# A fused attention and feed-forward kernel on one core: both products one item earlier, masks one item later, two row copies on ScalarE's queue

## What is computed

```python
for t in range(S):
    new_re = ar * S_re - ai * S_im
    new_im = ar * S_im + ai * S_re
    S_re, S_im = (new_re + kv, new_im)          # kv = outer(k_t, v_t)
    y[:, :, t] = einsum('bhd,bhde->bhe', q_t, S_re)
x = y as 3072 tokens of 384
h = x @ w_in;  x = (h * clip(h + 3, 0, 6) / 6) @ w_out          # 384 -> 2048 -> 384
h = x @ w_in2; out = (max(h, 0) + alpha * min(h, 0)) @ w_out2
```

## Time and profile before

| | |
|---|---|
| median of 3 runs (lowest, highest) | 1027.42 us (1025.89 to 1032.92) |
| the profiled execution: its time | 1026.65 us |
| its span, first to last instruction | 1024.7 us |
| mean granted TensorE clock | 0.986 of full speed |
| TensorE matmuls busy | 967.1 us, 94% of the span |
| VectorE busy | 599.4 us, 58% |
| ScalarE busy | 485.4 us, 47% |
| GpSimd busy | 263.2 us, 26% |

### The profile page before, as it was taken

One profiled execution on the slowest core, in us unless ns is written; L12 is line 12 of the kernel. 1 busy time (PEld: TensorE's weight loads), 2 busy tenths in 40 slices (PEclk: granted clock), 3 DMA queues, 4 the chain that ended last, 5 costly groups with the idle time before them and its releaser, 6 DMA issues.

```text
span 1024.7 us, 17083 instructions
## 1 busy us (share of the span) xinstructions
PE 967.1 (94%) x6498; PEld 869.2 (85%) x6498; DVE 599.4 (58%) x1088; ACT 485.4 (47%) x865; POOL 263.2 (26%) x235
## 2 busy tenths in 40 slices
PE   0799987999999999999999999999999999999997
PEld 0788877899999999999999998888888888888886
DVE  6767787778878878878772244453433433434332
ACT  7656666667677676777743453221221222212211
POOL 0000022222222222322222243333333333323332
PEclk9999988999999999999999999999999999999999
DMA  6752322333433333442221611001010010100000
GB/s 171 207 141 70 86 70 71 87 85 95 106 82 94 85 94 77 104 110 71 78 68 27 241 61 54 1 20 43 1 62 1 1 62 1 62 1 1 32 1 31
DMA packets 80930, 70.48 MB, mean 69 GB/s; under 512 B 32592, under 2 KB 78160, under 8 KB 80464
## 3 DMA queue, kind: packets, MB, share of 16 engines
q1 hardware_dynamic: 80208, 68.80, 24.7%
q10 hardware_dynamic: 640, 0.59, 0.3%
HBM read 40.90 MB, written 9.44 MB: 49 GB/s over the span
## 4 chain that ended last, share of the span: by engine, by line
PE 83%; SPq 5%; ACT 4%; DVE 4%; DMA 2%; issue 2%; DVEq 0%; ACTq 0%
PE op L1189 12%; PE op L1190 12%; PE hp L1190 12%; PE op L1191 12%; PE hp L1189 12%; PE hp L1191 11%; SPq L402 3%; PE yp L1177 3%; PE gp L1156 3%; SPq L405 2%; PE yp L1156 2%; DMA st<-prod 2%; PE gp L1184 2%; PE hp L1212 1%; PE tp L1165 1%
## 5 line engine op out<-in xcount | busy, mean ns | idle before, releaser
L524 POOL TENSOR_TENSOR g_lo<-gated,g_hi 128x384 fp32r<-128x384 f32 (+2 forms) x224 | 261.0, 1165 | 752.1 <-ACT g_hi L620 752.1
L620 ACT ACTIVATE g_hi<-gated 128x384 fp32r<-128x384 f32 (+2 forms) x224 | 123.3, 551 | 330.0 <-DVE gated L904 284.4
L900 DVE TENSOR_SCALAR gate<-hp,alpha_sb 128x512 f32<-128x512 f32 x96 | 72.1, 751 | 240.0 <-PE hp L1191 240.0
L889 DVE SCALAR_TENSOR_TENSOR gated<-gate,hp 128x384 f32<-128x384 f32 (+1 forms) x144 | 72.8, 506 | 125.3 <-ACT gate L613 125.0
L1189 PE MATMUL op<-g_hi,wb_hi 128*128 128x384 f32 (+1 forms) x384 | 129.3, 337 | 0.4 <-ACT out_sb L625 0.2
L1189 PE MATMUL hp<-x_hi,wa_hi 128*128 128x384 f32 (+1 forms) x384 | 126.0, 328 | 0.0
L613 ACT ACTIVATE gate<-hp,half 128x384 f32<-128x384 f32 (+1 forms) x144 | 77.2, 536 | 101.9 <-PE hp L1191 87.7
L1191 PE MATMUL op<-g_hi,wb_lo 128*128 128x384 f32 (+1 forms) x384 | 124.8, 325 | 0.0
L1190 PE MATMUL op<-g_lo,wb_hi 128*128 128x384 f32 (+1 forms) x384 | 124.7, 325 | 0.0
L1191 PE MATMUL hp<-x_hi,wa_lo 128*128 128x384 f32 (+1 forms) x384 | 123.7, 322 | 0.0
L1190 PE MATMUL hp<-x_lo,wa_hi 128*128 128x384 f32 (+1 forms) x384 | 123.6, 322 | 0.0
(11 more groups left out here) (110 smaller groups left out, 1704.1 us busy)
## 6 DMA issues: line engine op xcount, KB each, us to landing
st<-prod SPq DMA_DIRECT2D x92, 145.1 KB, 2.9
a_sb<-a_in SPq DMA_DIRECT2D x24, 288.0 KB, 4.0
qk_sb<-qk_in SPq DMA_DIRECT2D x24, 288.0 KB, 3.6
v_pad<-v_in SPq DMA_DIRECT2D x24, 192.0 KB, 3.8
x_raw<-x SPq DMA_DIRECT2D x6, 768.0 KB, 5.6
out<-out_sb SPq DMA_DIRECT2D x6, 768.0 KB, 4.0
st<-prod SPq DMA_DIRECT2D x96, 32.2 KB, 2.3
wa_raw<-w_in SPq DMA_DIRECT2D x6, 512.0 KB, 6.1
```

Of the source, the lines that this page charges most:

```text
L524: pool.tensor_tensor(g_lo[:, at, 0:wide], gated[:, at * UT:at * UT + wide], g_hi[:, at, 0:wide].bitcast(F32), ALU.subtract).then_inc(glo_d ...
L620: act.activation(g_hi[:, at, 0:wide], gated[:, at * UT:at * UT + wide], ACT.Copy).then_inc(ghi_done, 1)
L889: dve.scalar_tensor_tensor(out=gated[:, to], in0=gate[:, at], scalar=1.0, in1=hp[:, n % 2, 0:wide], op0=ALU.min, op1=ALU.mult).then_inc(ga ...
L900: dve.tensor_scalar(gate[:, at], hp[:, n % 2, 0:wide], 0.0, alpha_sb[:, m:m + 1], ALU.min, ALU.mult).then_inc(gate_done, 1)
```

## The change

The strings of the short slots change: `c` goes from the third item to the second, so that `forward` and `backward` stand together; `d` stays in the third and `e` and `g` join it from the fourth, so that both products stand in the third; `f` (masks) goes from the second item to the fourth, and `o` (outputs) from the third to the fourth, where `v` remains. `stack(c1)` on SyncE goes with `g` to the third item. For the chunks that a short slot prepares (and chunk 2), the two large row copies of the second product are issued on ScalarE's queue: in the fourth item, with `f`, behind `gate_of`, `copy_k` and `logs` of that item if it has them, and ahead of `inverses`. The function for this is there already, and serves chunks 0 and 1: it waits for `ends_set` and for the second product.

```diff
-SHORT = {6: ("a", "bf", "cdo", "egv", "hij", "kl"), 7: ("a", "bf", "cdo", "egv", "hi", "j", "kl")}
+SHORT = {6: ("a", "bc", "deg", "fov", "hij", "kl"), 7: ("a", "bc", "deg", "fov", "hi", "j", "kl")}
...
+def is_short(s):
+    return width(items_of(s)[-1] // MT_FF) == FIRST * CH
+
+def two_queues(c):
+    return c <= FIRST or is_short(c - 1)
...
# SyncE, in stack(c)
-                for to, rows in high_stack(c, 1) + ([] if c < FIRST else low_stack(c, 1)):
+                for to, rows in high_stack(c, 1) + ([] if two_queues(c) else low_stack(c, 1)):
...
# ScalarE, ahead of the loop over items
             inverses(3)
+            stack(2)
             gate_of(0)
...
# ScalarE, in the loop over items
+                if "f" in steps and c1 is not None and two_queues(c1):
+                    stack(c1)
                 if "v" in steps and c2 is not None:
                     inverses(c2)
```

More of the change, by code:

```diff
@@ L126, in places @@
         items = items_of(s)
-        plan = (SHORT if width(items[-1] // MT_FF) == FIRST * CH else LONG)[len(items)]
+        plan = (SHORT if is_short(s) else LONG)[len(items)]
         for steps, n in zip(plan, items):
```

## The result

| | before | changed |
|---|---|---|
| median | 1029.99 us (4 runs, 1025.89 to 1032.92) | 1039.65 us (4 runs, 1039.17 to 1042.63) |
| profiled execution, its span | 1026.65, 1024.7 us | 1039.17, 1037.5 us |
| mean granted clock | 0.986 | 0.984 |

The ratio (of the means; the medians differ by 9.7 us) is 1.0103, 95% interval 1.0056 to 1.015: slower by about 10.6 us. The forecast was no change, 1027.0 in a range from 1016 to 1036, with a chance of 0.1 for slower; it missed.

A forecast was written before the change was run, and what follows sets the result against it. TensorE's stops and low clock in slots 2 to 8 were taken as the bound: 143.8 us of work, 22.8 of stops and 7.5 of clock make 174.1 against 174.5, hence 1027.0 us, range 1016 to 1036.

The forecast's parts named there:

- The wait moves from the copies to the masks: Slots 2 to 8: TensorE stops mid-slot for VectorE's masks, about 2.2 us seven times, instead of for row copies.
- The wait for `leave` in slot 4: Slot 4, third item: TensorE's `output(16)` waits 2.5 us for `leave`, which now stands behind logs.
- The split that `high` feeds: Behind ScalarE's issues: TensorE wants this split two items later, so the delay costs nothing in slots without weight splits.
- VectorE's lag: VectorE starts phases behind TensorE's scores: 1 us on slots 3 to 5, 3 us on slot 6, 4 us in all.
- The clock: Slots 2 to 8: five of seven stops each cost 1.7 us of low clock, 8.5 less 1 hidden: 7.5 us.
- Rival B: The clock holds through the 2.2 us stops: less 7.5 us, 1019.5 us, chance 0.2.
- The start of slot 2: Ahead of item 0, ScalarE's `stack(2)` delays nothing: 0, bound 0 to 1.2 us.
- ScalarE's issues in slots with splits: Fourth item: two issues on ScalarE, 1.25 us a pair, would cost 1.25 to 3 us a slot without cover.
- Rival C: ScalarE's fourth-item wait and issues hold up VectorE's split and carry its lag over: 8 to 10 us, 1036 us, chance 0.14.
- phases more than 0.2 us behind the scores: Sign of Rival C at slot starts: VectorE starting phases this late delays ScalarE's waves and the second item's gate.
- The sum: Slots 2 to 8: work 143.8, stops 22.8 and clock 7.5 make 174.1 us against 174.5, no change.
- the signs named beforehand: Next profile: mask waits seven times, `leave` wait, PEclk 0.93 in most slots, slots 4 and 5 shorter, slot 8 longer.

The follow-up runs named there:

- e3: The changed kernel with the masks moved back to the second item, behind backward: 1025.52 us, ratio 0.9978 to the kernel before.
- e10: The kernel before with only masks, outputs and new_state moved to the fourth item, all copies on SyncE: 1045.47 us, ratio 1.0172.
- e11: The kernel before with backward and logs in the second item, both products in the third, all copies on SyncE: 1022.22 us, ratio 0.9945.
- e1: The changed kernel's order alone, with SyncE issuing all 12 row copies: 1041.6 us, ratio 1.0124 to the kernel before.
- e12: The changed kernel with ScalarE's two issues in the fifth item and chunk 2 all from SyncE: 1040.84 us, ratio 1.0126 to the kernel before.
- e5: e3 without the second queue, all twelve row copies on SyncE: 1020.4 us, ratio 0.9911 to the kernel before.
- e6: e3 with chunk 2's copies all issued from SyncE, without `stack(2)` on ScalarE: 1027.01 us, ratio 0.9976 to the kernel before.
- e2: The kernel before, order kept, with the two copies on ScalarE's queue in the fourth item, chunk 2's too: 1036.55 us, ratio 1.0081.

## Why the prediction was wrong, step by step

**The wait moves from the copies to the masks: right, its size partly by luck.** Forecast 16.3 us at the masks (2.3, 2.3, 1.4, 3.7 and three of 2.2); measured 16.0, with none in slot 4 and 2.95 in slot 3. In slot 8 both sides of the sum were late and the difference held: the masks ended 15.2 us behind the slot's start instead of 13.7, and TensorE arrived after 12.9 us instead of 11.4, most of it by the stop for `g_lo`. The copies left the path. That the masks are the harm is shown by e3 and e10, that the products' half is a gain by e11. The wait for `leave` in slot 4 was forecast at 2.5 and came out at 2.5.

**The stops for `g_lo`, 7.4 us, had no term: wrong.** The sentence "The split that `high` feeds is wanted by TensorE two items later ... so this is nothing" looked only at the high part of the fourth item, and of that it was right (e1 and e12 against the change). The one of the second item had been put behind logs and the table load by the same edit. By the prediction's own rows it had nothing to spare in slot 8: 3.1 us from the second copy of keys (218.5) to `high` and 1.2 from there to the end of `g_lo` (an estimate from the slot of before, 221.09, 224.19 and 225.40) is 222.8, and TensorE wants it at 222.68.

**VectorE's lag: wrong.** Forecast 1 us on slots 3 to 5 together, 3 us on slot 6, none behind, 4 us of stops in all; measured 1.6 to 3.2 us in slots 3 to 6 and still 1.36 and 1.35 in slots 7 and 8. It showed up in the stops for `g_lo`, which were 1.32 and 1.34 us in slots 7 and 8. Both are needed for these: with logs in the same place and a lag of 0.15 and 0.30 us, e5 stops for `g_lo` by nothing and 0.18 us in these two slots; with a lag of 1.35 us in both but logs in the third item, e10 does not stop for it there. Slot 8 of e5, TensorE and VectorE, then of e10:

```profile
206.74 1.16 PE L1168 MATMUL gp<-st 96*128 96x128 f32 x8 [0.89 <-DMA st<-prod]
207.04 1.70 DVE L802 TENSOR_TENSOR_SCAN t_phase<-ones,t_frac,t_dt 128x128 f32<-128x128 f32 x3
216.14 0.39 PE L1201 MATMUL op<-g_hi,wb_hi 128*128 128x256 f32 x1 [0.18 <-POOL g_lo L534]
```

```profile
228.59 1.05 PE L1168 MATMUL gp<-st 96*128 96x128 f32 x8
229.94 1.71 DVE L802 TENSOR_TENSOR_SCAN t_phase<-ones,t_frac,t_dt 128x128 f32<-128x128 f32 x3
```

Why VectorE is late without any wait of ScalarE (e1, e12) is argued, not shown: TensorE's stop at the head of a slot, in which VectorE used to catch up, is gone. Stops in all: 22.8 forecast, 26.7 measured; 7.4 for `g_lo` and 0.8 for VectorE's gate came in, the 4 of the lag fell out.

**The clock: the largest miss.** I took 1.7 us for each of five stops, less 1, which is 7.5; the profile gives 13.8. The price of a stop that I drew from the earlier trace rows, 1.7 us for one near 2.2 us, does not hold: 2.16 and 2.95 us cost nothing in slots 2 and 3, while slots 6 and 8 lost 3.4 us each, and slot 7, with nearly the stops of slot 8, lost 1.7. What decides between them is not shown. The low clock also varies from run to run: e12, one program, spans 1032.4 us at a mean clock of 0.993 and 1041.5 us at 0.98. In the first of these, its profiled execution, the slots take 179.1 us with 28.3 us of stops, which leaves 7.0 for the clock, about what I had forecast for the change. Taken alone, more stops (+6.2), the late start and what lies behind slot 8 make +9.2 us on 1027.4, which is 1036.6 and already just past the edge of the range; the clock's +3.6 carries it further. Rival B did not come about: the clock fell in five of the seven slots, in slots 4, 6, 7 and 8 with no single stop above 2.5 us. The Trainium skill's page "TensorE: Matmul & The Clock Gate", section "Why this matters for your kernels", which stood beside rival B, warns only of idle gaps above about 3 us; this trace disagrees.

**The start of slot 2.** I gave `stack(2)` 0, bound 0 to 1.2; slot 2 was 1.9 us late, but e6 is late without it. So the term itself is not shown to be wrong; the sum lacked one for a start that differs between programs, whose cause is open.

**ScalarE's issues in slots with splits, "1.25 to 3 us a slot" if uncovered: right as a mechanism, wrong about where.** In the order before it costs 8 us (e2), with masks second 0.67% (e3 against e5), in the changed order nothing (e1 and e12 against the change). Rival C named this as the way to 1036. Its sign, phases more than 0.2 us behind the scores, came true in slots 3 to 8, but its cause did not: e1 has the same lag without ScalarE's wait. The time came by the masks, `g_lo` and the clock. Why it hides there is argued, not shown: in slot 8 ScalarE is through with its issues at 234.33 and TensorE is held by the masks until 234.48.

**The sum.** Forecast 174.1 for the slots, measured 184.3: stops +3.9, clock +6.3. With the start +1.9 and what lies behind slot 8 +1.1, the profiled execution comes to 1039.5 instead of 1026.3 (measured 1039.2). The median of the three runs that the prediction had, 1027.42, became 1029.99 with a fourth, so the ratio is a little lower than these numbers. Of the signs named beforehand, the waits for the masks, for `leave` and the longer slot 8 came; PEclk 0.93 in most slots did not (1.00 twice, 0.86 to 0.88 four times), and slot 5 grew by 0.6 us instead of getting shorter.

## What to carry over

A wait at the head of a round can be the cover under which something else is late, as VectorE's round was here: before an operation is put behind others, look for the instruction on the bounding engine that reads it, and do so for every result of every item that is moved, the side results too. Put a transfer's issue on a compute engine's queue only where what it waits for is long done: the same two issues gained 0.8% an item later and lost 0.8% an item earlier. Count the stops of TensorE with a range for the clock behind them, since stops of 2.2 to 2.95 us cost between nothing and 3.4 us here.

## What the hardware showed unexpectedly

TensorE's granted clock stayed at 2.4 GHz through stops of 2.16 and 2.95 us in two slots, and was at 1.2 GHz for 6.8 us after 1.34 and 2.38 us within slot 8 and for 3.4 us after 1.32 and 2.38 us within slot 7. One and the same program (e12) ran at mean clocks of 0.98 to 0.993, with spans 9.1 us apart.
